# A two-layer MLP on one core: another order for nine sets of prepared weights, and earlier stores of ScalarE's weights

## What is computed

```python
def _moe_ref(x, w_in, w_out):            # 3072 tokens, 512 -> 2048 -> 512
    h = x @ w_in
    g = np.where(h > 0.0, h, np.exp(np.minimum(h, 0.0)) - 1.0)
    return (g @ w_out).astype(np.float32)

def _moe2_ref(x, w_in, w_out, s, b):
    r = np.maximum(x @ w_in, 0.0)
    g = s * (r * r) + b
    return (g @ w_out).astype(np.float32)

def reference(...):
    x = attention(q, k, v, mem_k, mem_v) as [3072, 512]
    return _moe2_ref(_moe_ref(x, ...), ...)
```

## Time and profile before

| | |
|---|---|
| median of three runs | 1146.09 us |
| the profiled execution's own time | 1145.91 us |
| its span (first to last instruction) | 1143.9 us |
| TensorE busy | 1098.1 us (96%) |
| VectorE busy | 822.1 us (72%) |
| ScalarE busy | 781.3 us (68%) |
| GpSimd busy | 389.7 us (34%) |
| mean granted TensorE clock | 0.989 |

### The profile page before, as it was taken

How to read it: one execution, slowest core, us unless ns; L and a number is a source line. 1 busy time by engine, 2 the same in 40 slices (tenths; PEclk the granted TensorE clock), 3 DMA queues, 4 the chain that set the end, 5 groups by cost and what they waited for, 6 DMA issues and landing times.

```text
span 1143.9 us, 18152 instructions
## 1 busy us (share of the span) xinstructions
PE 1098.1 (96%) x5787; PEld 876.1 (77%) x5787; DVE 822.1 (72%) x1210; ACT 781.3 (68%) x1842; POOL 389.7 (34%) x427
## 2 busy tenths in 40 slices
PE   8999898979999999989999999999999999999998
PEld 4667666757767778878788787888888888888886
DVE  5796686458886965898877968868848568576475
ACT  4797686667658757758758678667677476774574
POOL 5789689741232432136276113663000000000000
PEclk9999999989999999999999999999999999999999
DMA  9998999989889989869899789898697666776664
GB/s 202 268 273 254 345 330 354 348 268 323 251 237 251 269 256 263 280 210 348 301 358 348 233 263 373 300 349 282 186 282 233 189 198 189 219 218 193 194 192 158
DMA packets 204054, 302.80 MB, mean 265 GB/s; under 512 B 112824, under 2 KB 121016, under 8 KB 203960
## 3 DMA queue, kind: packets, MB, share of 16 engines
q1 hardware_dynamic: 203960, 301.65, 85.4%
HBM read 226.10 MB, written 75.50 MB: 264 GB/s over the span
## 4 chain that ended last, share of the span: by engine, by line
PE 73%; ACT 6%; DMA 6%; DVE 5%; issue 4%; POOL 3%; SPq 3%; ACTq 0%; POOLq 0%; DVEq 0%
PE ps L1020 35%; PE ps L1005 31%; DMA w_scratch<-w_new 3%; ACT ps L1100 2%; PE ps L914 2%; DMA w_ring<-w_scratch 1%; DVE g_lo L1494 1%; PE ps L939 1%; POOL w_new L801 1%; PE ps L966 1%; POOL att L801 1%; ACT elu L1193 1%; PE ps L923 1%; PE ps L908 1%; DVE nbias L1347 1%
## 5 line engine op out<-in xcount | busy, mean ns | idle before, releaser
L1005 PE MATMUL ps<-xc_hi,w_ring 128*128 128x512 f32 x1344 | 435.9, 397 | 5.0 <-ACT s L1166 3.7
L1020 PE MATMUL ps<-g_hi,w_ring 128*128 128x512 f32 x1344 | 420.4, 394 | 11.4 <-issue 6.4
L1005 PEld LDWEIGHTS ps<-xc_hi,w_ring 128*128 128x128 f32 x1344 | 253.9, 189 | 63.8 <-issue 4.0
L1020 PEld LDWEIGHTS ps<-g_hi,w_ring 128*128 128x128 f32 x1344 | 249.9, 189 | 68.3 <-issue 9.0
L1005 PE MATMUL ps<-xc_lo,w_ring 128*128 128x512 f32 x672 | 263.2, 392 | 0.0
L1020 PE MATMUL ps<-g_lo,w_ring 128*128 128x512 f32 x672 | 263.1, 392 | 0.0
L801 POOL TENSOR_TENSOR w_new<-w_raw,w_new 128x256 fp32r<-128x256 f32 x179 | 165.9, 933 | 219.0 <-ACT w_new L1247 215.8
L1494 DVE TENSOR_TENSOR g_lo<-X,g_hi 128x512 fp32r<-128x512 f32 x240 | 178.4, 748 | 30.5 <-ACT g_hi L1233 30.0
L1233 ACT ACTIVATE g_hi<-X 128x512 fp32r<-128x512 f32 x240 | 150.1, 629 | 56.8 <-PE ps L1020 55.1
L1020 PEld LDWEIGHTS ps<-g_lo,w_ring 128*128 128x128 f32 x672 | 126.7, 189 | 26.9
L1005 PEld LDWEIGHTS ps<-xc_lo,w_ring 128*128 128x128 f32 x672 | 127.2, 189 | 24.4
(11 more groups left out here) (125 smaller groups left out, 1350.5 us busy)
## 6 DMA issues: line engine op xcount, KB each, us to landing
w_ring<-w_scratch SPq DMA_DIRECT2D x336, 512.0 KB, 4.4
w_scratch<-w_new SPq DMA_DIRECT2D x179, 256.0 KB, 5.3
w_scratch<-att SPq DMA_DIRECT2D x45, 256.0 KB, 4.8
w_raw<-in_moe_w_in SPq DMA_DIRECT2D x16, 512.0 KB, 5.6
w_raw<-in_moe_w_out SPq DMA_DIRECT2D x16, 512.0 KB, 6.0
x_scratch<-y SPq DMA_DIRECT2D x12, 512.0 KB, 6.1
att<-x_scratch SPq DMA_DIRECT2D x12, 512.0 KB, 5.9
out<-elu SPq DMA_DIRECT2D x24, 256.0 KB, 4.3
```

What stands on the lines that cost most here:

```text
L1005: last = nc.tensor.matmul(bank_of(st, st.i), w[:, a, cols], x[:, st.pi, kk, :], start=(st.pi in (P1, P5) and kk == 0 and n == 0), stop=(kk ...
L1020: last = nc.tensor.matmul(bank_of(st, d), w[:, a, cols], x[:, k % RING, :], start=(st.pi in (P1, P5) + (P4,) * (1 - st.gr) and st.i == 0 a ...
```

## The change

Two things. First, for sets 5 to 13 alone, the products are made in the order P1, P4, P2, P7, P5, P6, P3 in place of P1, P4, P7, P2, P5, P6, P3, on ScalarE and SyncE, and GpSimd makes sums 2, 3 and 4 in one go after P2's low part. Before, its order was: sum 1, P1, P4, sum 2, sum 3, P7, P2, P5, P6, sum 4, P3. Now it is: sum 1, P1, P4, P2, sum 2, sum 3, sum 4, P7, P5, P6, P3. Second, for all products from 35 on, the store of a product cut at step `at` is due in iteration `(at + 1) // 2 + 3` in place of `at // 2 + 4`. For an odd `at` that is the same iteration, for an even `at` it is one iteration (two steps) sooner.

```diff
+SUMS_FIRST = (P1, P4, P2, P7, P5, P6, P3)
...
+def sums_first(ms):
+    return len(ms) == 1 and 5 <= ms[0] < PAIR
+
+
 def order_of(ms):
+    if sums_first(ms):
+        return [(ms[0], pi) for pi in SUMS_FIRST]
     return [(m, pi) for m in ms for pi in PREPARED[:2]] + [(m, pi) for pi in PREPARED[2:] for m in ms]
...
-    return early if early < HEAD_PREP else HEAD_PREP + sum(at // 2 + 4 <= d for at in HI_SLOT.values())
+    return early if early < HEAD_PREP else HEAD_PREP + sum((at + 1) // 2 + 3 <= d for at in HI_SLOT.values())
...
                     for pi in (P1, P4):
                         split_w(m, pi)
+                if sums_first(ms):
+                    split_w(ms[0], P2)
                 for m, (a11, a12, a21, a22) in zip(ms, blocks):
                     pool.wait_ge(w_sums, sums_count(m, 1))
                     nc.gpsimd.tensor_tensor(a22, a22, a21, ALU.subtract).then_inc(w_sums, 1)
                 for m, (a11, a12, a21, a22) in zip(ms, blocks):
                     pool.wait_ge(w_sums, sums_count(m, 2))
                     nc.gpsimd.tensor_tensor(a11, a22, a11, ALU.add).then_inc(w_sums, 1)
+                if sums_first(ms):
+                    a11, a12, a21, a22 = blocks[0]
+                    nc.gpsimd.tensor_tensor(a12, a12, a22, ALU.subtract).then_inc(w_sums, 1)
+                    for pi in (P7, P5, P6, P3):
+                        split_w(ms[0], pi)
+                    return
```

## The result

The changed kernel takes 1149.61 us (median of 12 runs, 1143.29 to 1153.04), the kernel before beside it 1145.8 us (12 runs, 1142.57 to 1149.76): a ratio of 1.0035, with an interval from 1.0019 to 1.0052. So it is slower by some 4 us. The prediction was 2.9 us less. The time lies inside the range, but on the other side of the kernel before. Two executions of all that follow, of 3817 and of 1227 us, were disturbed and stand in no ratio.

A forecast was written before the change was run, and what follows sets the result against it. The prediction took the kernel to be bound by TensorE, with gains in 100 to 250 us. Its terms, 5.6 + 2.1 - 1.0 - 3.8 = 2.9 us less than 1145.9, gave 1143.0 us, range 1136 to 1151.

The forecast's parts named there:

- The new order, TensorE's side: Sets 6, 8 and end of set 10: TensorE's gaps and one half clock go, 5.6 us won (0.8 to 9).
- The named gaps: TensorE's waits traced to the fourth sum, sets 6 to 10: 1.40 and 0.33, 0.44, 1.34, 2.06 us, to go.
- ScalarE's waits for sums: Sets 5 to 13: about 9 us of some 21 stay, moved from P3's cut to P5's.
- the gap of step 43: Set 9, at 184.5 us: 1.34 us goes, but the 0.35 us wait at 173.5 grows by 1.6: zero.
- the gap of step 45: End of set 10, 191 us: TensorE waits 0.3 in place of 2.06 us, half clock (1.7) goes: 3.5 us.
- the second rival: Sets 5 to 13: P5's wait costs TensorE what P3's did, some 3 us more, 1149 us; chance 0.14.
- The port, taken at nothing: VectorE and GpSimd sharing an SBUF port: GpSimd's instruction count stays, so nothing was taken for it.
- The raw load of set 15: First layer, TensorE's 4.43 us wait: load leaves 2.1 us sooner, 2.1 us won, 1.7 more at the upper end.
- Ring loads, first layer: Loads queued behind stores not ready: three reach TensorE by 0.2 to 0.4 us, 1.0 us lost together (0 to 3).
- Ring loads, second layer: Sooner stores delay loads, clearest at P7 of set 21 and 707 us: 3.8 us lost (1.6 to 8.9).
- SyncE's queue decides: Both layers: landing times stay, full load delay shows, 6.3 us more, 1152 us; chance 0.14.
- the 1.7 us for halved clock: Second layer, after the 2.1 us gap at P7 of set 21: half clock follows, costing 1.7 us.

The follow-up runs named there:

- after: The changed kernel, both parts of the change, against the kernel before; its profiled execution took 1143.29 us, its median 1149.61 us, ratio 1.0035.
- once more: A second execution of the same kernel, nothing changed: the changed kernel 1151.87 us (1.0067), the kernel before 1144.5 us.
- before: The kernel without the change, as profiled for the prediction (1145.9 us); median 1145.8 us beside the changed kernel.

## Why the prediction was wrong, point by point

**The sum closes, with one term wrong.** By timed ratios, at 1145 us: the order alone +0.5 us (predicted -5.6); product 97's store sooner, under the new order, 0.9985 - 1.0004, -2.2 us, and under the old -3.6 (predicted -2.1); the other early stores of the first layer, 0.9993 - 0.9985, +0.9 us (predicted +1.0); the second layer +5.0 us, the 3.9 of the ten stores and the 1.1 of the others (predicted +3.8). Together +4.2 us, and +4.0 is measured. Each of these differences carries nearly 3 us either way, and the changed kernel itself was measured at 1.0035 and at 1.0067, so that the parts meet the whole this closely is luck; what holds is the order's own ratio, whose interval, -1.6 to +2.4 us, leaves no room for a gain of 5.6. The step that failed is "The new order, TensorE's side": it counted the gaps behind the cuts of sets 6, 8 and 10, and the half clock after one of them, as 5.6 us won, and the runs show +0.5 us, since as much idle time comes up at other steps of the first tile. With zero there, the rest of the prediction would have given 2.7 us more than before.

**The named gaps went, and others came.** The copies and products that waited for the fourth sum no longer do. Near 141 us TensorE waits 0.50 us in after where it waited 1.40 (but 1.77 in after once more), and where it waited 1.34 at set 9's end (step 43) and 2.06 at set 10's (step 45) it waits 0.51 and 0.62, the last line below. Timeline of after, ScalarE and then TensorE:

```profile
170.86 0.42 ACT L1262 ACTIVATE att<-w_raw 128x256 fp32r<-128x256 f32 x1 [2.42 <-POOL w_raw L824]
171.18 0.47 ACT L1106 ACTIVATE att<-ps 128x384 f32<-128x384 f32 x1
```

```profile
140.03 0.55 PE L911 MATMUL ps<-ident,att 96*128 96x96 f32 x4 [0.50 <-ACT att L1135]
...
171.71 0.63 PE L923 MATMUL ps<-may_see,chunk_of 3*96 3x512 bf16 x2 [0.81 <-ACT att L1106]
...
187.05 0.73 PE L1035 MATMUL ps<-g_hi,w_ring 128*128 128x512 f32 x2 [0.62 <-DVE g_lo L1509]
```

Neither the gap at 191 us nor the halved clock at 194 is there. ScalarE's waits for sums were 8.0 us with the order alone, where 9 were forecast (4.4 of the 8.0 lie behind 330 us, and some at P5 are told as "issue"). But at P5 they do reach TensorE: in after ScalarE stands 2.42 us for the third sum of set 9, the copy (L1106) comes right behind that cut, and TensorE waits 0.81 us for it at step 36, where it waited 0.35. All nine traces of the new order have this wait, 0.6 to 1.7 us. The prediction had seen the place, let the wait grow by 1.6 us and set the gap of step 43 against it; the gap of step 45, worth 3.5 of the 5.6 us with its half clock, was there in half of the old order's traces only. So the second rival, a wait that only changes its name at P5, came near the outcome (1149), and its mechanism is there, if at one place and smaller than P3's wait.

At step 32 the gap grew by about 1.7 us, as much as step 33 lost: the two together take 3.2 us on average in either order, and the runs that change set 8 alone keep this sum within 1 us (2.98 against 0.91 + 1.97; 1.80 + 1.99 against 2.80). After has halved stretches of 3.4 us at 161 and 216 us. Four comparisons of new against old order under equal stores give +0.5 us (the order alone), +1.6 (1.0067 against 1.0053), +1.8 (0.9985 against 0.9969) and +1.1 us (0.9974 against 0.9964), the last two measured on different chips. What is shown is that the gain is zero or slightly less, and that TensorE's idle time moves between steps of the first tile and doesn't shrink, 20.3 us on average in both. What holds the sum constant, a chain through VectorE, GpSimd and the DMAs, is only argued and stays open.

**A sum over one trace.** The 5.6 us were added from gaps and halved stretches of a single execution, and its first tile was one of the slow ones, 3.6 us longer than the next trace of the same kernel. Its halved stretches in the first tile, four with 17.1 us in all, were treated as consequences of single waits; the other five traces of the old order have 3.4 to 10.2 us. Their place differs too: the gap of set 10's end was followed by half clock in before (2.06 us) and once more (2.04 us), and by full clock in the old order with product 97 sooner, though it is longest there (2.73 us). A gap or a stretch that another execution doesn't have is no gain.

**The port, taken at nothing.** "The number of GpSimd's instructions stays, so I take nothing for it" was wrong in its reason. The number stays, but they now come without pauses, beside VectorE's two-input instructions. Over 1 to 319 us VectorE's mean instruction takes 695 to 709 ns in the nine traces with the new order, 684 to 696 ns in six with the old one: some 4 us over 330 instructions. It is real, and by the runs on set 8 it isn't the price of the order.

**The raw load of set 15: right.** It left sooner as forecast, and TensorE's wait at step 70 fell by 2.4 us on average. The timed gain is 3.6 us in the old order and 2.2 in the new, where 2.1, or 3.8 at the upper end, was the term. It is the one part whose gain is clear of noise (0.9969 [0.9951, 0.9987]).

**Ring loads, first layer: the waits came, their price is within the noise.** The +0.9 us timed is as good as zero or 3, so that it meets the term of 1.0 shows nothing. After has the waits that were to be looked for, 2.9 us in the first tile (5.2 once more), the longest at step 58, where the order alone, with the stores as before, has 2.51 us for ScalarE's copy in its place:

```profile
214.22 0.50 PE L1020 MATMUL ps<-xc_hi,w_ring 128*128 128x512 f32 x1 [2.43 <-DMA w_ring<-w_scratch]
```

Under the old order the same early stores seem to cost more: all stores sooner is 1.0053, 6.1 us, of which some 5 are the second layer's, so that they give back all of product 97's 3.6 us. Its first tile has 6.4 us of waits for ring loads, where product 97 alone has 1.7. Why the order matters to them is open: SyncE's waits for low parts don't tell it.

**Ring loads, second layer: right in mechanism, wrong in two details that nearly cancel.** The store of P7 of set 21 did move ahead of the load, TensorE's gap at 547 us is 2.22 us (2 to 3 forecast), and TensorE loses 0.43 us at step 304 and, one tile later, 0.49 to 0.79 us at steps 360, 362 and 364 (1 us forecast at 707). The six of the ten stores that move, moved alone, reproduce it, and without them it is all but gone. But I took 0.9 us of delay on the ground that the backlog of the DMAs would drain while the load waits to be issued. For these loads it did not: issued 1.9 us later against TensorE's steps, the load of step 252 took 8.94 us to land where it took 8.56, and that of step 364, issued 1.5 us later, 8.07 where it took 7.54 (8.28 against 8.11, and 8.89 against 8.88, once more). Two loads ahead it did in part: the load of step 246, issued 1.75 us later, took 4.36 us in place of 5.39 (4.85 in place of 6.21). The loads of steps 246 and 248 both went out later too, 1.75 and 2.7 us, behind the stores of products 145 and 146, so the queue that the third load met had moved with it. The full delay shows at the last load, as the rival "SyncE's queue decides" had it: TensorE's waits at steps 248 to 252 grow by 1.9 us (1.6 once more), where 0.9 was the term, and at 360 to 364 by 1.7 (1.8), where it was 0.9. Against that, the 1.7 us for halved clock never came, after 2.22 us or any other of these gaps. The two mistakes cancel, so that 3.8 us comes near the measured cost is partly luck. Seven loads were late where five were forecast, with 5.4 us of waiting against 1.3 before (5.3 against 1.7 once more); from step 200 on the trace is 4.8 us longer, where 3.8 was the term. The Trainium skill, in "DMA: Bandwidth & Descriptors", section "Queues, rings and completion order", has descriptors consumed in ring order within a queue. No run here tests it by itself: the landing times above don't speak against it, but the loads were late by their issue already.

**What beats both kernels.** The old order with product 97's store one iteration sooner and the six of the second layer one later: 1140.41 us, 0.9964 [0.9946, 0.9981]. Product 97 alone is as good within the noise.

## What to carry to other kernels

In an in-order queue that carries both stores and prefetches, a store let out before its data is ready delays the prefetches behind it (here six such stores cost 3.9 us); let out early the one store that something waits for (3.6 us gained), and keep the others behind the prefetches where those have no slack. An idle gap is a gain only where a second trace of the same kernel shows it too: here two executions differed by 3.6 us in the stretch from which 5.6 us were to come, and the gap worth most was there in half of the traces. Count the idle time of the whole stretch, not of the gap alone: the new order emptied two gaps and filled others, and the sum stayed at 20.3 us. Taking a handshake off an engine moves its wait to the next resource (here from sums to slots: 21.3 us became 8.0, and 19.6 became 36.3), so ask what is late next before any of it is counted.

## What the runs showed of the hardware

VectorE's two-input instruction of 128x512 takes 0.68 us alone and 1.20 us while GpSimd's subtractions of 128x256 follow each other; GpSimd's take 1.18 us each at that place and 0.74 alone. In the old order the loser at the same place is GpSimd alone, as the kernel before shows at the place of the fences above:

```profile
160.40 4.62 POOL L801 TENSOR_TENSOR att<-w_raw,att 128x256 fp32r<-128x256 f32 x2 [0.68 <-ACT att L1247]
...
160.80 0.68 DVE L1489 TENSOR_TENSOR X<-X 128x512 f32<-128x512 f32 x1
```

Its two subtractions last 4.62 us while VectorE keeps 0.68 us. The Trainium skill says in "SBUF — State Buffer", section "Who interferes with whom", that the two hold a shared port against each other and the loser is wholly blocked. The second case agrees; in the first both are slowed, to some 1.2 us each, and one instruction of each goes by every 1.13 us; whether they block each other in turn or share can't be told from the lengths. A ring load that was issued 2 us later into a backlog, with the loads ahead of it late as well, did not land in less time (8.94 against 8.56 us; 8.28 against 8.11 once more). And a gap of TensorE of 2.22 us at 545 us was followed by full clock, as one of 2.73 us that ended at 192 us was in the old order with product 97 sooner, where one of 2.06 us in the earlier trace rows was followed by half clock.
